# Who issues the loads of v in a woven attention and feed-forward kernel: SyncE, or GpSimd from the ninth pair on

## What is computed

```python
attn = softmax(scale * q_c @ k_c.T)          # 9 chunks of 64, each within itself
x = (attn @ v_c) as [4608, 512]
x = x / rms(x) * rms_g
h = silu(x @ w_gate) * (x @ w_val)           # 512 -> 1536
y = h @ w_out                                # 1536 -> 512
u = (y @ w_in2) * clip(y @ w_in2 + 3, 0, 6) / 6   # 512 -> 2048
out = u @ w_out2                             # 2048 -> 512
```

## Time and profile before

| | before |
|---|---|
| median of three runs | 1652.73 us (1647.89 to 1653.22) |
| the profiled execution, its own time | 1651.29 us |
| its span | 1649.5 us |
| mean granted clock of TensorE | 0.996 |
| TensorE, VectorE, ScalarE, GpSimd busy | 97%, 64%, 52%, 48% |
| chain that ended last | 85% TensorE |

### The profile page before, as it was taken

One profiled execution on the slowest core, in us unless ns is written; L12 is line 12 of the kernel. 1 busy time (PEld: TensorE's weight loads), 2 busy tenths in 40 slices (PEclk: granted clock), 3 DMA queues, 4 the chain that ended last, 5 costly groups with the idle time before them and its releaser, 6 DMA issues.

```text
span 1649.5 us, 29728 instructions
## 1 busy us (share of the span) xinstructions
PE 1605.6 (97%) x11335; PEld 1569.5 (95%) x11337; DVE 1047.5 (64%) x1441; ACT 858.5 (52%) x1341; POOL 786.9 (48%) x772
## 2 busy tenths in 40 slices
PE   7889999999999999999999999999999999999998
PEld 5678999899999999999999999999999999999998
DVE  4878877868754556655554776665666765455454
ACT  4666766655544444544444665555655644434432
POOL 2543543449786654434340376777676630231231
PEclk9999999999999999999999999999999999999999
DMA  9577777554566555989997856656658986776674
GB/s 177 133 170 184 176 201 173 143 159 155 167 229 208 195 205 184 366 311 310 311 316 275 304 210 238 210 183 246 227 189 274 372 275 204 220 230 210 212 227 119
DMA packets 335646, 366.88 MB, mean 222 GB/s; under 512 B 186256, under 2 KB 299152, under 8 KB 332304
## 3 DMA queue, kind: packets, MB, share of 16 engines
q1 hardware_dynamic: 321584, 334.69, 64.3%
q0 software_dynamic: 8800, 28.85, 5.1%
q10 hardware_dynamic: 5120, 1.44, 0.5%
HBM read 200.80 MB, written 164.10 MB: 221 GB/s over the span
## 4 chain that ended last, share of the span: by engine, by line
PE 85%; DVE 3%; issue 3%; ACT 2%; DMA 2%; POOL 2%; SPq 2%; ACTq 0%; DVEq 0%; POOLq 0%
PE bx L968 14%; PE by L968 14%; PE bx L970 13%; PE by L970 13%; PE bx L969 13%; PE by L969 13%; DMA hl_b<-h_scratch 1%; SPq L568 1%; PE att L937 1%; PE att L946 1%; PE att L895 1%; DMA hl_d<-u_scratch 1%; PE att L918 1%; DVE wr L1511 1%; DVE tx L1498 1%
## 5 line engine op out<-in xcount | busy, mean ns | idle before, releaser
L968 PE MATMUL by<-tx,wr 128*128 128x384 f32 x840 | 286.2, 341 | 2.7 <-ACT vb L1176 1.0
L968 PE MATMUL bx<-tx,wr 128*128 128x384 f32 x840 | 285.8, 340 | 2.7 <-ACT gb L1176 1.2
L970 PE MATMUL bx<-tx,wr 128*128 128x384 f32 x840 | 281.4, 335 | 0.0
L970 PE MATMUL by<-tx,wr 128*128 128x384 f32 x840 | 281.3, 335 | 0.0
L969 PE MATMUL by<-tx,wr 128*128 128x384 f32 x840 | 281.2, 335 | 0.0
L969 PE MATMUL bx<-tx,wr 128*128 128x384 f32 x840 | 281.2, 335 | 0.0
L1549 DVE TENSOR_TENSOR hl_d<-hl_d 128x1536 fp32r<-128x1536 f32 x84 | 146.2, 1774 | 94.0 <-ACT hl_d L1248 93.9
L1867 POOL DMA_DIRECT2D out_dram<-ot x128 | 70.2, 556 | 248.3 <-DVE ot L1572 245.8
L1549 DVE TENSOR_TENSOR hl_b<-hl_b 128x1152 fp32r<-128x1152 f32 x84 | 118.9, 1431 | 106.1 <-ACT hl_b L1248 105.3
L1248 ACT ACTIVATE hl_d<-hl_d 128x1536 fp32r<-128x1536 f32 x84 | 123.3, 1486 | 113.7 <-DMA hl_d<-u_scratch 113.4
L968 PEld LDWEIGHTS by<-tx,wr 128*128 128x128 f32 x840 | 158.0, 188 | 7.2 <-DVE ub L1523 1.9
(11 more groups left out here) (193 smaller groups left out, 3773.3 us busy)
## 6 DMA issues: line engine op xcount, KB each, us to landing
hl_d<-u_scratch SPq DMA_DIRECT2D x84, 768.0 KB, 4.4
hl_b<-h_scratch SPq DMA_DIRECT2D x84, 576.0 KB, 5.7
u_scratch<-ut SPq DMA_DIRECT2D x48, 576.0 KB, 3.7
h_scratch<-ht SPq DMA_DIRECT2D x36, 576.0 KB, 3.6
u_scratch<-ub SPq DMA_DIRECT2D x96, 192.0 KB, 2.8
u_scratch<-ub SPq DMA_DIRECT2D x48, 384.0 KB, 2.5
h_scratch<-vb SPq DMA_DIRECT2D x72, 192.0 KB, 3.5
h_scratch<-vb SPq DMA_DIRECT2D x36, 384.0 KB, 3.1
```

Source lines behind the costliest of these rows:

```text
L968: pe.matmul(dst, w_hi, m_hi, start=start, stop=False, skip_group_check=not opens)
L970: return pe.matmul(dst, w_lo, m_hi, start=False, stop=stop, skip_group_check=not opens)
```

## The change

It leaves all work on the other engines in its order. `load_v(7)` stays with SyncE. `load_v(8)` to `load_v(35)`, 28 pairs and 56 DMAs, go to GpSimd, with the same wait for `attn_done`, into the same slot AT + 1 of the pair before; there they stand behind an x sum of the first step (`FIRST_SUMS`) and ahead of everything else of the slot. Their DMAs count on a semaphore of their own, for which the attends from pair 8 on wait.

```diff
+    v_loaded_late = sem("v_loaded_late")
...
                 n = woven(m, slot, AT, 1)
-                if n is not None and n + 1 < NN:
-                    load_v(n + 1)
+                if n == NG:
+                    load_v(NG + 1)
...
-                pe.wait_ge(v_loaded, 32 * (n - NG + 1))
+                pe.wait_ge(*((v_loaded, 32 * (n - NG + 1)) if n < NG + 2 else (v_loaded_late, 32 * (n - NG - 1))))
...
+        def load_v(n):
+            t, p = tp_of(n)
+            pool.wait_ge(attn_done, n)
+            for e in range(2):
+                pool.dma_start(v_a[e * CH:(e + 1) * CH, :, 0:DH],
+                             v[2 * p:2 * p + 2].rearrange("c (j e) s d -> e s (c j) d", e=2)[e, t * CH:(t + 1) * CH]).then_inc(v_loaded_late, 16)
...
                 if m == 0 and slot in FIRST_SUMS:
                     x_sum(0, FIRST_SUMS[slot])
+                n = woven(m, slot, AT, 1)
+                if n is not None and NG < n < NN - 1:
+                    load_v(n + 1)
                 n = woven(m, slot, AT, 2)
                 if n is not None:
                     inverse_rms(n)
```

## The result

The changed kernel takes **1677.51 us** (median of four runs, 1675.2 to 1678.94) against 1652.78 for the kernel before in the same comparison: a ratio of **1.0153**, 95% interval 1.014 to 1.0166, so 25 us slower. The forecast was 1654.3 us with a range up to 1660. The profiled execution has 1676.42 us (span 1674.6), 25.1 more than that of before.

What follows compares the result with a forecast made beforehand. TensorE, busy 97%, was taken as the bound, so only its idle time at 50 to 350 us counts. Terms 0.2 - 0.8 + 1.7 + 1.7 + 0.2 = +3.0 us on 1651.29 gave 1654.3 us, range 1647.0 to 1660.0.

Steps and rivals of the forecast that it cites:

- (a): Pair 7's slot: step 0's weight sums 3.8 us later; TensorE loses 1.5, wins 0.69 at pair 8; 0.2 to 0.4 left.
- (b): Pair 9's slot: load_v(10) delays inverse_rms(9), TensorE waits 1.5 us more; +0.2 us left at 120 us.
- (c): Pair 12's attend: of its 3.44 us wait TensorE gains 0.8; the rest becomes waits on pair 13's probabilities.
- (d): Steps 5, 8, 11: x sums behind slot 8's load, 2.4 us late in step 8; TensorE loses 1.7, 1.7, 0.2 us.
- (e): All other slots: GpSimd idling or later slack covers the loads, costing nothing unless a pair exceeds about 2 us.
- Rival 2: Nothing is covered: at 1.9 us a pair, steps 5, 8 and 11 cost 2.8 each; 1659.1 us; chance 0.14.
- Rival 3: Each GpSimd issue waits for a VectorE instruction of 0.7 us; a pair costs 2.9; 1658.5 us, or 1665; chance 0.05.
- Rival 1: GpSimd's issues hide; TensorE keeps all three v waits and the earlier k, 5.6 us; 1645.7 us; chance 0.16.

Runs made afterwards that it cites:

- three powers: Kernel before, SyncE issuing every v; GpSimd waits for the same attend and runs three unused one-column powers in the slots of loads 19, 25, 31: 1658.33 us, ratio 1.0037.
- without the three loads: Changed kernel, but SyncE issues v of pairs 19, 25 and 31 and GpSimd keeps the other 25 pairs: 1651.79 us, ratio 0.9992.

## Why the prediction was wrong

**Right: the price and the early waits.** A pair costs 1.40 us (1.5 forecast), landing 4.1 (3.3). Pairs 8 and 12 have no issue wait. Pair 13's probabilities get a wait of 1.71 us (2 to 2.5 forecast).

**Mis-sized: (a), (b) and (c), with errors that cancel.** Both waits of (a) and (b) came, 1.22 us at pair 7's x and 2.28 in place of 1.41 at pair 9's. I let the later waits absorb them and kept +0.2. A profile is one execution, and here one isn't enough: nine kernels have the same program as the kernel before up to pair 18 (itself among them), and from pair 6 to pair 18 they come between 0.7 us earlier and 3.8 later than it, 1.4 later on average. Four kernels have the early program of the change. The averages of the two groups:

| us lost against the profiled kernel before | pairs 6 to 11 | 11 to 18 | 6 to 18 |
|---|---|---|---|
| nine with SyncE's loads (6 to 18: from -0.7 to 3.8) | 0.7 | 0.8 | 1.4 |
| four with the change's loads (6 to 18: from 1.2 to 2.0) | 2.1 | -0.7 | 1.4 |

So (a) and (b) cost about 1.4 us and not 0.2, and (c) brought about 1.5 and not 0.8. Together they come to nothing, where I had -0.6. That the sum comes near is luck, and the differences between single kernels of either group are larger than the terms.

**Failed: (d).** I followed GpSimd's delay of 2.4 us through ScalarE to its copy for the attend and left VectorE out. Its fill of x stands between the second sum and the eviction that the same attend waits for, and in the profile of before that eviction had less to spare than the copy: it ended at 248.08, 0.4 us ahead of the attend.

```profile
246.54 0.94 DVE L1498 TENSOR_TENSOR tx<-xt,tx 128x768 fp32r<-128x768 f32 x1
247.40 0.68 DVE L1492 TENSOR_TENSOR xr<-att,g_col 128x512 f32<-128x512 f32 x1
```

Two parts were missed:

- *Lateness alone*, with VectorE let in (three powers): 3.5, 2.1 and 2.0 us in steps 5, 8 and 11 where I had 1.7, 1.7 and 0.2. The wait is for VectorE's eviction and not for the copy, and in steps 5 and 11 the slower clock behind it is included (1.5 and 1.4 us). Some 1 us of step 5 isn't lateness: five kernels that leave these x sums as they were come 0.8 to 1.1 us later there than the profiled kernel before.
- *The lock-out.* Steps 5, 8 and 11 of the changed kernel cost 7.5, 7.5 and 4.8; less the above 4.0, 5.4 and 2.9, or **12.3 us**, 2.4 of them by the slower clock behind the longer waits. The profile of before had the evidence: the third sum at 244.08 took 2.58 us where 1.83 is usual, while a fill ran. So the two engines were already in each other's way there, though that row alone doesn't tell that a DMA would keep VectorE out of three sums. I read this stretch for who waits for whom and not for instructions that took longer than their kind. *The Trainium skill, "SBUF — State Buffer", section "Who interferes with whom", says that a VectorE instruction with two SBUF inputs contends with a GpSimd one that reads SBUF, and that who issues first has the ports for its whole instruction. The trace agrees for a single sum, with the fill's end 0.82 us behind it. By that rule the fill of the changed kernel would have ended behind the second sum, after 2.2 us; behind a DMA of GpSimd it ended behind the fourth, after 5.8.*

**Failed: (e), "all other slots: nothing".** The stall of 5.13 us made 4.6 at pair 23. No row of before showed it: GpSimd issued no DMA in that stretch. My bounds for the price went by DMAs that were issued one at a time and never asked whether it holds for the 32nd.

**The sum again**, from the runs: late at pair 18 +0.8; lateness 3.5 + 2.1 + 2.0; lock-out 12.3; stall 4.6; together 25.3 us, measured 25.5 at pair 35. All of these are against the one profiled execution of before; the medians are 24.7 us apart.

**Rivals.** Rival 2 had the right place (steps 5, 8, 11) and too small a price, 2.8 us a step. Rival 3 had VectorE holding GpSimd's issues; it was the other way round. The 56 issues took 684 to 845 ns. *By the rule of the Trainium skill, "SBUF — State Buffer", section "SBUF: two separate sides", that I weighed they would have taken some 3100 beside a two-port instruction; no issue of this kernel shows that.* Rival 1 fell with (a), (b) and (c): even without the three loads, and with the stall where it costs nothing, the kernel gained nothing that can be told (0.9976 to 1.0008).

## What to carry to other kernels

Before moving work to an engine, look for pairs of engines whose instructions already stretch each other (a sum of 2.58 us among sums of 1.83), and follow a delay through both. A DMA issued on GpSimd can matter beyond its issue: keep it away from stretches where GpSimd runs long SBUF instructions back to back beside VectorE instructions with two SBUF operands, or leave just those loads on SyncE (three of 28 here, worth 18 us by the medians). Before you price a freed wait at its full length, look at what stands right behind it: of 3.44 us TensorE kept 0.4 by one profile and about 1.5 by the averages. And don't read half a microsecond off one profile: over the same 130 us of program nine profiles here are up to 4.5 us apart.

## What the runs showed of the hardware that I had not expected

- While a GpSimd sum of 128x768 runs, VectorE's fill makes no progress: in all kernels a fill that was held ended 0.80 to 0.86 us behind the sum that held it, whether that was one sum, two or three (2.2, 4.0, 5.8 us).
- If VectorE gets in between two such sums, the second takes up to 2.6 us and not 1.8. Whether it gets in depends, in steps 5, 8 and 11, on a DMA that GpSimd issued just before its sums: behind one it was kept out in 17 of the 18 steps where at least two of these sums stood back to back behind the load (six kernels), without one never. Ahead of a one-column power it got in behind a DMA too.
- Issuing many runs on GpSimd stalled it once in the woven stretch, 3.0 to 5.2 us between the 31st and 32nd load of 512 runs in all seven kernels that issue so many whole ones, whatever the place in the program.
- Of three in a row, a one-column subtraction takes GpSimd 0.16 us and a one-column power 0.53.
